# A fused attention, gated MLP and mixer kernel: tails transposed together, first loads on two queues, key sums moved up in each step

## The reference

```python
# attention with exponential features, per batch and head
def phi(x):
    proj = x @ w_phi                                   # 64 -> 128
    proj = proj - max(abs(proj), over features)
    return concat(exp(proj), exp(-proj))               # 256 features
kv  = phi(k).T @ v            # 256 x 64, a sum over all 576 keys
z   = sum over keys of phi(k)
out = (phi(q) @ kv) / (phi(q) @ z + 1e-6)
x   = heads side by side: 4 x 576 x 512
# gated MLP
h   = relu(x @ w_in)                                   # 512 -> 1024
c   = convolution of h over the sequence, 3 taps
x   = (h * sigmoid(c)) @ w_out                         # 1024 -> 512
# mixer
u   = x + (U V applied along the sequence, rank 32)
out = u + relu(u @ w_ch1) @ w_ch2                      # 512 -> 2048 -> 512
```

## Time and profile before

| | |
|---|---|
| median of 3 runs | 932.11 us (931.59 to 932.53) |
| the profiled execution | 931.04 us |
| its span, first to last instruction | 929.2 us |
| PE busy | 900.5 us, 97% |
| DVE, ACT, POOL busy | 377.8, 326.5, 90.9 us |
| granted TensorE clock, mean | 0.995 |

### The profile page before, as it was taken

How to read it: one execution, slowest core, us unless ns; L and a number is a source line. 1 busy time by engine, 2 the same in 40 slices (tenths; PEclk the granted TensorE clock), 3 DMA queues, 4 the chain that set the end, 5 groups by cost and what they waited for, 6 DMA issues and landing times.

```text
span 929.2 us, 14087 instructions
## 1 busy us (share of the span) xinstructions
PE 900.5 (97%) x5752; PEld 834.3 (90%) x5752; DVE 377.8 (41%) x655; ACT 326.5 (35%) x621; POOL 90.9 (10%) x60
## 2 busy tenths in 40 slices
PE   6899999999999999999998999999999999999997
PEld 4667889887988889889998999999999999999997
DVE  5455477226774355652595543221211122122111
ACT  5665565334653444543443332111211211211111
POOL 3323022000120001110042001010010010010000
PEclk9899999999999999999999999999999999999999
DMA  7986641304722236114356540110200300300101
GB/s 177 265 229 159 195 143 39 114 17 152 225 51 65 77 102 228 46 46 160 114 191 201 168 124 20 57 46 1 73 30 1 100 3 2 101 1 23 47 1 34
DMA packets 106032, 88.91 MB, mean 96 GB/s; under 512 B 61041, under 2 KB 92657, under 8 KB 103921
## 3 DMA queue, kind: packets, MB, share of 16 engines
q1 hardware_dynamic: 105968, 88.02, 31.6%
HBM read 70.18 MB, written 17.83 MB: 95 GB/s over the span
## 4 chain that ended last, share of the span: by engine, by line
PE 85%; DVE 4%; SPq 4%; DMA 3%; issue 2%; ACT 1%; ACTq 0%
PE qnb L1067 7%; PE qnb L1069 7%; PE qnb L1068 7%; PE qnb L1163 7%; PE mb L1067 6%; PE kvb L1124 6%; PE pjb L1067 5%; PE mb L1069 5%; PE mb L1068 5%; PE pjb L1069 5%; PE pjb L1068 5%; PE tpb L1067 2%; PE kvb L1069 2%; PE kvb L1067 2%; PE tpb L1068 2%
## 5 line engine op out<-in xcount | busy, mean ns | idle before, releaser
L985 DVE SCALAR_TENSOR_TENSOR c_lo<-qnb,c_hi 128x384 fp32r<-128x384 f32 x94 | 52.4, 558 | 284.9 <-ACT c_hi L752 284.9
L752 ACT ACTIVATE c_hi<-qnb 128x384 fp32r<-128x384 f32 x94 | 46.3, 492 | 296.6 <-PE qnb L1069 296.6
L1067 PE MATMUL qnb<-u_hi,w_b 128*128 128x384 f32 x384 | 129.8, 338 | 0.0
L1069 PE MATMUL qnb<-u_hi,w_b 128*128 128x384 f32 x384 | 128.4, 334 | 0.0
L1068 PE MATMUL qnb<-u_lo,w_b 128*128 128x384 f32 x384 | 128.4, 334 | 0.0
L809 DVE TENSOR_REDUCE nm<-pjb 128x4 f32<-128x512 f32 (+1 forms) x80 | 50.7, 633 | 84.5 <-PE pjb L1069 84.3
L508 POOL TENSOR_TENSOR g_lo<-cv,g_hi 128x576 fp32r<-128x576 f32 x32 | 48.2, 1505 | 361.5 <-DVE g_hi L794 361.5
L1067 PE MATMUL mb<-x_hi,winr 128*128 128x288 f32 x224 | 72.3, 323 | 0.1
L1067 PEld LDWEIGHTS qnb<-u_hi,w_b 128*128 128x128 f32 x384 | 72.1, 188 | 0.1
L1068 PEld LDWEIGHTS qnb<-u_lo,w_b 128*128 128x128 f32 x384 | 72.1, 188 | 0.0
L1069 PEld LDWEIGHTS qnb<-u_hi,w_b 128*128 128x128 f32 x384 | 72.1, 188 | 0.0
(11 more groups left out here) (257 smaller groups left out, 1929.2 us busy)
## 6 DMA issues: line engine op xcount, KB each, us to landing
winr<-wi_dram SPq DMA_DIRECT2D x32, 512.0 KB, 4.6
woutr<-wo_dram SPq DMA_DIRECT2D x15, 1024.0 KB, 5.9
stage<-in_moe_w_ch_dram SPq DMA_DIRECT2D x32, 256.0 KB, 4.6
us<-u_dram SPq DMA_DIRECT2D x6, 768.0 KB, 4.7
ua<-u_dram SPq DMA_DIRECT2D x6, 768.0 KB, 4.8
kr<-in_k_dram SPq DMA_DIRECT2D x32, 128.0 KB, 3.0
qr<-in_q_dram SPq DMA_DIRECT2D x32, 128.0 KB, 2.7
vt<-in_v_dram SPq DMA_DIRECT2D x32, 128.0 KB, 2.9
```

Of the source, the lines that this page charges most:

```text
L752: nc.scalar.activation(c_hi[:, j % CR, :], CH[j % 2][:, 0:TW], ACT.Relu).then_inc(s_chh, 1)
L985: nc.vector.scalar_tensor_tensor(out=c_lo[:, j % CR, :], in0=CH[j % 2][:, 0:TW], scalar=0.0, in1=c_hi[:, j % CR, :].bitcast(F32), op0=ALU. ...
L1067: mm(o, a_hi, b_hi, start=start, stop=False)
L1069: return mm(o, a_lo, b_hi, start=False, stop=stop)
```

## The change

1. The transposes of a tail move from step 5g - 1 to 5g - 3 (`T_TAIL`), and the transpose of the result's tail of pair g - 3 (`TAILS` = 3) goes into the same use of `TP`, in other columns: "p" is gone as a use of its own. A period has four uses ("q", "t", "k", "o") and one step without. ACT and DVE make both copies in one visit, with one count. Step -3 is now the first, and the tail of pair 0 the first use.
2. The first loads: SP issues q's tail, one half of k, both halves of q; ACT issues k's tail, the other half of k and both copies of w_phi, ahead of its first activation. The loads of q no longer stand behind SP's wait for the zeroed v.
3. The weight block c = 2 of the output product is loaded at m = 12 of SP's list where it was at m = 13.
4. PE: `contract_k` stands ahead of MLP piece 0, and `project` ahead of `kv_by_feature`. ACT: `key_values` stands ahead of `prepare_high`.
5. In batch 3 the low part of the last gated block is made by DVE, not POOL, with a semaphore of its own.
6. The first loads of u for the last product are issued among the loads of w_in of batch 3, and no longer wait for the store of batch 2's u.
7. `hidden2(1, 2)` stands ahead of the wait for the last four additions into u.

```diff
-    T_K, T_TAIL, T_Q, T_OUT, T_OUTT = -2, -1, 1, 10, 12
+    T_K, T_TAIL, T_Q, T_OUT, T_OUTT = -2, -3, 1, 10, 12
+    TAILS = (T_OUTT - T_TAIL) // PERIOD
...
     def tp_use(tick):
-        for kind, offset in (("o", T_OUT), ("q", T_Q), ("p", T_OUTT), ("k", T_K), ("t", T_TAIL)):
-            if here(tick, offset) is not None and (kind, here(tick, offset)) != ("p", NP - 1):
+        for kind, offset in (("o", T_OUT), ("q", T_Q), ("k", T_K)):
+            if here(tick, offset) is not None:
                 return kind, here(tick, offset)
-        return None
+        n, i = divmod(tick - T_TAIL, PERIOD)
+        return ("t", n) if i == 0 and 0 <= n < NP - 1 + TAILS else None
...
@@ SP, ahead of its list @@
-            load_k(0)
+            load_tail(0, QROWS, qd)
+            load_k(0, 0)
             for h in range(2):
-                sp.dma_start(ph_raw[h * D:(h + 1) * D, :], w_phi).then_inc(s_phi_ld, 16)
-            load_tail(0)
+                load_q(0, h)
             sp.wait_ge(s_zero, 2)
-            load_q(0)
             load_v(0)
...
@@ SP, weights @@
-                    if m in (13, 14):
-                        load_wout(b, m - 11)
+                    if m in (12, 14):
+                        load_wout(b, m // 2 - 4)
...
@@ SP, behind its list @@
             for j in range(WR, J1):
                 load_win(B - 1, j)
+                if j == J1 - 3:
+                    sp.wait_ge(s_xl, len(TPN))
+                    sp.wait_ge(s_ust, 16 * (B - 2))
+                    load_u(us, s_us, 0)
+                    load_u(ua, s_ua, 0)
             sp.wait_ge(s_u, 2 * CC * (B - 1))
             sp.dma_start(u_dram[:, :, (B - 2) * S:(B - 1) * S], x1[:, :, :]).then_inc(s_ust, 16)
-            sp.wait_ge(s_xl, len(TPN))
-            sp.wait_ge(s_ust, 16 * (B - 1))
-            load_u(us, s_us, 0)
-            load_u(ua, s_ua, 0)
...
@@ POOL @@
-            for n in range(J1 * B):
+            for n in range(J1 * B - 1):
                 gate_low(n)
...
@@ ACT, copies of the transposes @@
                 if kind == "t":
-                    act.wait_ge(s_pj, max(0, PERIOD * (g - 1) + TL + 1))
-                    copy(xl_hi[:, :], TP[:, 0:P]).then_inc(s_xh, 1)
+                    if g < NP:
+                        act.wait_ge(s_pj, max(0, PERIOD * (g - 1) + TL + 1))
+                        last = copy(xl_hi[:, :], TP[:, 0:P])
+                    if g >= TAILS:
+                        last = copy(x0_hi[:, (g - TAILS) % XS, MAIN:S], TP[:, P:P + TAIL])
+                    last.then_inc(s_xh, 1)
...
@@ ACT, ahead of its first activation @@
+            act.dma_start(tl[KROWS, 0, :, :],
+                          kd[0, 0, :, MAIN:S, :].rearrange("h s d -> s h d")).then_inc(s_tld[0], 16)
+            act.dma_start(kr[:, 0, :, 1, :],
+                          kd[0, 0, 1, 0:MAIN, :].rearrange("(p t) d -> p t d", t=TM)).then_inc(s_kld[0], 16)
+            for h in range(2):
+                act.dma_start(ph_raw[h * D:(h + 1) * D, :], w_phi).then_inc(s_phi_ld, 16)
             act.wait_ge(s_ident, 1)
...
@@ ACT, in a step @@
                 mlp(b, m, 1)
+                g = here(tick, 4)
+                if g is not None:
+                    key_values(g)
                 for n in range(NA):
                     if tick == prep_tick(n):
                         prepare_high(n)
-                g = here(tick, 4)
-                if g is not None:
-                    key_values(g)
...
@@ DVE, batch 3 @@
                     gate_high(b, j - 1)
+                if j == J1:
+                    dve.wait_ge(s_gh, J1 * B)
+                    sub(g_lo[:, J1 - 1, :], cv[:, (J1 * B - 1) % HR, :],
+                        g_hi[:, J1 - 1, :].bitcast(F32)).then_inc(s_glast, 1)
...
@@ PE, in a step @@
-                mlp(b, m, 0)
                 g, u = unit_at(tick - 2)
                 if g is not None and u <= TL:
                     contract_k(g, u)
+                mlp(b, m, 0)
                 mlp(b, m, 1)
-                g = here(tick, KVT0)
-                if g is not None:
-                    kv_by_feature(g)
                 g, u = unit_at(tick)
                 if g is not None:
                     if tick == 0:
                         pe.wait_ge(s_phi, 2)
                     project(g, u)
+                g = here(tick, KVT0)
+                if g is not None:
+                    kv_by_feature(g)
                 use = tp_use(tick)
...
@@ PE, ahead of the last product @@
+            hidden2(1, 2)
             pe.wait_ge(s_u, 2 * CC * B)
             for j in range(J2):
-                if j > 1:
+                if j > 2:
                     hidden2(1, j)
```

More of the change, by code:

```diff
@@ L57, in program @@
     MLP0 = PERIOD * (PAIRS - 1) + T_OUTT + 1
-    FIRST = T_K
+    FIRST = T_TAIL
     END = PERIOD * (NP - 1) + CQ0 + 2
@@ L109, in x0_use @@
     def x0_use(b):
-        return TPN["p" if b < B - 1 else "o", PAIRS * b + PAIRS - 1]
+        last = PAIRS * b + PAIRS - 1
+        return TPN["t", last + TAILS] if b < B - 1 else TPN["o", last]
     OUTS = [(c, h) for c in range(CC) for h in range(2)]
@@ L311, in _, with load_k, load_tail, load_q @@
                 sp.sem_inc(ahead, count)
[L313 to L329, removed]
+            def load_k(g, h):
+                sp.dma_start(kr[:, g % 2, :, h, :],
+                             kd[g // PAIRS, g % PAIRS, h, 0:MAIN, :].rearrange("(p t) d -> p t d", t=TM)
+                             ).then_inc(s_kld[g % 2], 16)
+            def load_tail(g, rows, src):
+                sp.dma_start(tl[rows, g % 2, :, :],
+                             src[g // PAIRS, g % PAIRS, :, MAIN:S, :].rearrange("h s d -> s h d")
+                             ).then_inc(s_tld[g % 2], 16)
+            def load_q(g, h):
+                sp.dma_start(qr[:, g % 2, :, h, :],
+                             qd[g // PAIRS, g % PAIRS, h, 0:MAIN, :].rearrange("(t p) d -> p t d", p=P)
+                             ).then_inc(s_qld[g % 2], 16)
             def load_v(g):
@@ L392, in _ @@
             sp.dma_start(cw[:, :, :], conv_w.rearrange("k (p j) -> p k j", j=J1)).then_inc(s_const_ld, 16)
-            load_k(1)
-            load_tail(1)
-            load_q(1)
+            for h in range(2):
+                load_k(1, h)
+            load_tail(1, QROWS, qd)
+            load_tail(1, KROWS, kd)
+            for h in range(2):
+                load_q(1, h)
             load_v(1)
@@ L412, in _ @@
                     sp.wait_ge(s_tp, TPN["k", g] + 1)
-                    load_k(g + 2)
+                    for h in range(2):
+                        load_k(g + 2, h)
                 g = here(tick - 1, T_TAIL)
@@ L416, in _ @@
                     sp.wait_ge(s_tp, TPN["t", g] + 1)
-                    load_tail(g + 2)
+                    load_tail(g + 2, QROWS, qd)
+                    load_tail(g + 2, KROWS, kd)
                 g = here(tick - 1, T_Q)
@@ L420, in _ @@
                     sp.wait_ge(s_tp, TPN["q", g] + 1)
-                    load_q(g + 2)
+                    for h in range(2):
+                        load_q(g + 2, h)
                 g = here(tick - 1, 4)
@@ L599, in transposed_high @@
                     last.then_inc(s_xh, 1)
-                if kind == "p":
-                    copy(x0_hi[:, g % XS, MAIN:S], TP[:, 0:TAIL]).then_inc(s_xh, 1)
             def query_features(g, half):
@@ L1083, in transposes @@
                 if kind == "t":
-                    pe.wait_ge(s_tld[g % 2], 32 * (g // 2 + 1))
-                    last = nc.tensor.transpose(TP[:, 0:P], tl[:, g % 2, :, :].rearrange("p h d -> p (h d)"),
-                                               ident[:, :])
+                    if g < NP:
+                        pe.wait_ge(s_tld[g % 2], 32 * (g // 2 + 1))
+                        last = nc.tensor.transpose(TP[:, 0:P], tl[:, g % 2, :, :].rearrange("p h d -> p (h d)"),
+                                                   ident[:, :])
+                    if g >= TAILS:
+                        last = nc.tensor.transpose(TP[:, P:P + TAIL], at[QROWS, (g - TAILS) % 2, TM, :],
+                                                   ident[QROWS, QROWS])
                 if kind == "o":
@@ L1093, in transposes @@
                         last = nc.tensor.transpose(KVT[:, 0:TAIL], at[QROWS, g % 2, TM, :], ident[QROWS, QROWS])
-                if kind == "p":
-                    last = nc.tensor.transpose(TP[:, 0:TAIL], at[QROWS, g % 2, TM, :], ident[QROWS, QROWS])
                 last.then_inc(s_tp, 1)
@@ L1197, in outputs @@
                         pe.wait_ge(s_wo[c % 2], woutr_loads(b, c))
-                if e == 0:
+                if e == 0 and (b, last) == (B - 1, J1):
+                    pe.wait_ge(s_gl, J1 * B - 1)
+                    pe.wait_ge(s_glast, 1)
+                elif e == 0:
                     pe.wait_ge(s_gl, J1 * b + last)
```

28 lines of the change are left out of this document (16 added, 12 removed).

## The result

The changed kernel takes 921.29 us as a median of 4 runs (919.92 to 921.39), the kernel before 931.85 beside it (930.87 to 932.53): a ratio of 0.9884, with a 95% interval from 0.9867 to 0.9901. The forecast was 920.2 with a range of 916.0 to 925.5. The profiled execution took 919.92 us, its span is 918.1; against the 929.2 of before that is 11.1 us less, where 11.85 was forecast. The other three runs are 1.4 us longer, at a mean clock of 0.997 or 0.998 where the profiled one had 0.999; what that may be is said at the end.

What follows compares the result with a forecast made beforehand. TensorE (PE) was taken as the bound, 85% of the chain of waits, with gains in its pauses and half-speed stretches. Terms summed to -11.85 us, 932.11 to 920.3; forecast 920.2, range 916.0 to 925.5.

Steps and rivals of the forecast that it cites:

- Part 4: Pair 1's period: copying key sums before ACT's split ends the 2.5 us wait, -4.5 us; PE's `project` swap, -0.5.
- Part 2: The start: k's transposes wait for DVE's split of w_phi, first projection at 9.5 instead of 7.97; +1.85 us in all.
- 0.45 for another operand: Start, step 3: ACT copies pair 1's tail only after a w_in split, delaying DVE's tail-feature difference, +0.45 us.
- Part 1: Tails sharing a bank use: PE's wait on k's low part goes; -1.8 us attention alone, -0.6 and -0.7 MLP stage.
- Part 3: Weight block c = 2 of the output product, loaded one step earlier, lands before its use: -2.4 us.
- Part 5: `contract_k` ahead of MLP piece 0 on PE: order alone gives 0 us (-0.4 to +0.4).
- Cover: MLP stage: without piece 0's 1.77 us in between, K0's features keep 0.57 us of margin; priced at 0.
- Part 6: End of batch 3: waits for the low part (-0.6), last weight block (-1.7) and additions (-0.9) go; -3.2 us together.

Runs made afterwards that it cites:

- b_load: The kernel before with only the first loads issued as in the changed kernel, every order the old one: 924.69 us beside 930.62.
- u_kv: The changed kernel with `key_values` back behind `prepare_high` on ACT: 918.40 us beside 931.21 for the kernel before.
- b_order: The kernel before with `contract_k` ahead of MLP piece 0 on PE as its one edit: 931.13 us beside 930.53.
- s_phi: The changed kernel with ACT issuing both copies of w_phi first, ahead of k's tail and half of k: 918.99 us beside 930.62 for the kernel before.
- u_wout: The changed kernel with weight block c = 2 of the output product loaded at m = 13 again: 924.96 us beside 930.62 for the kernel before.
- u_order: The changed kernel with `contract_k` back behind MLP piece 0 on PE: 919.47 us beside 931.21 for the kernel before.
- u_end: The changed kernel with the three edits at the end of batch 3 undone: 924.20 us beside 931.21 for the kernel before.
- best3: The changed kernel with `contract_k` behind piece 0, pair 0's tail low part ahead of w_phi's split, pair 1's loads ahead of U, V: 918.26 us beside 930.62.

## Why the prediction came out as it did

The time was right, and every wait that was to go went. One cause was wrong, its number right by luck, and the start was mis-sized.

**Part 4, the step that failed.** It forecast -4.5 us for pair 1's period from `key_values` ahead of `prepare_high` ("Now the copy goes first"). The period did fall by 4.47, but another edit does that alone. The first loads alone (b_load) take 4.9 us off that period with the old order, by a store that lands 3.1 us sooner; with them in, the new order gives nothing and costs 0.9 of the period (16.84 us against 15.96 in u_kv) and 0.6 in pair 0. The prediction held the piece it needed, "the store also goes out some 4 us earlier, since SP is ahead by 2.5 us", but as a side effect: it didn't ask what ACT's 2.99 us of idle time would be after that, and shorter queues on SP were priced at 0.15 us in part 2. Its bound of -2.3 to -5.2 was also made for one cause; two edits that would both remove the same wait should have been priced one at a time. Some of the 21.3 us was also the clock of that one execution: the same code took 19.94 in b_order. The 0.7 us by which the split holds up the query features was right at 42 us (a wait of 0.7); the same thing at 25 us, a wait of 1.4, was seen in part 2 only as 0.45 for another operand. The early `project`, as cover for `kv_by_feature`, was not tried alone, and neither was the sharing of the bank's use (part 1).

**Part 2, mis-sized.** +1.85 forecast, +2.86 measured: k's transposes at 7.69 (6.9), first projection at 10.31 (9.5), so 0.8 by w_phi, and the rest by the wait at 25 us. w_phi's two loads, issued at 2.27 and 2.96 on ACT, take 3.2 us to land where they took 2.3 to 2.6 on SP's queue alone, while loads of k and q are under way from SP; in s_phi, issued first, they take 2.1. This is what the Trainium skill states (DMA: Bandwidth & Descriptors, Issuing engines are not separate DMA queues): the second queue saves issue time, and the loads share the engines and interleave. The trace is in line with it, with 0.6 and 0.8 us more for the two loads; the prediction guessed 1 us from the rule and set it aside for want of a row. The place in a queue counts all the same: moving w_phi ahead won 0.9 us.

**Part 1.** Three periods of 0.6: -1.27 measured for pairs 2 to 4. L1172 waits 0.28 for the division (`at`) in each, as forecast. 0.88 less 0.28 is the forecast 0.6, and 0.42 a period came; the 0.18 between wasn't traced to an instruction. In the MLP stage the gains of parts 1 and 4 (forecast -0.6, -0.7 and -0.5) came to -1.1 in all, by the table's steps without those of part 3, one of the three losses of part 5 in it; in the mixing the waits of 0.56 of the tail are replaced by waits of L1240 on DVE, 1.1 us in two, so there next to nothing was won.

**Part 3.** -2.4 forecast, -2.5 measured (-1.44 and -1.02, two of the three losses of part 5 in them), by u_wout even more; b_load shows that 1.1 of the 2.4 us of waits would have gone by the loads alone.

**Part 5.** 0 (-0.4 to +0.4) forecast; the order costs 0.68 over the three batches by u_order against the profile after; the 0.6 between the medians of b_order can't be told from none. Cover was not the matter: K0's features are on time in every step. What the prediction didn't look at is the bank of the output product: with two pieces back to back the 1.5 us of key sums no longer lie between them while ACT empties it. That loses 0.27 in each of three batches, enough for all of it.

**Part 6.** -3.2 forecast; 0.77, 1.94 and 1.22 us at the three places, 3.9 in sum, and 4.05 when undone. Each was the size of its wait plus 0.1 to 0.3 of refill.

In sum: the start, part 1 and the MLP stage brought 1.0, 0.5 and 0.7 us less than forecast, the end 1.4 more (0.7 of that behind the last product, in the last store of the output, which comes with the first loads by b_load). The total is within 0.75 us of the profile because these cancel.

## What to carry to other kernels

When two edits could each remove the same wait, price each with the other undone; here the cheap one (four loads fewer at the head of a queue) did it alone, and with it in the visible reorder cost time. A shorter issue queue is worth what its latest consumer waits for: follow each wait on a DMA back to its issue, and from there up the queue to the start. A long piece of background work is best put in the time in which its engine would wait anyway, here even ahead of work with a nearer due time.

## What the hardware showed beyond expectation

- A pause of PE of 1.4 us around 25 us is followed by half clock in some executions and not in others. In the profiles of u_order and u_wout the stretch behind it (26 to 29.5 us) is at 0.50 to 0.66; in those of the changed kernel, u_end and s_phi it is at 1.00. The changed kernel's runs fall into 919.92 at a mean clock of 0.999 and three of 921.3 at 0.997 and 0.998, while u_kv, whose pause there is 0.6 us, has four runs within 0.25 us. best3, with the same pause, has two runs at 917.35 and 917.87 (0.999 and more) and two at 918.65 and 918.68 (0.998). That these belong together is argued from two profiles and the run clocks, not shown run by run.
- The 2.5 us wait of before cost 2.5 and, behind it, about as much again by the clock: b_load takes 4.9 us off the period with one edit. In b_order, the same code there, the wait was 2.0, the granted clock of the 6.7 us window 0.76 in place of 0.50, and the period 1.4 shorter. A wait of 1.9 us in u_wout cost 3.6.
- A 32 KB load of w_phi lands 2.1 to 2.2 us after its issue when it is first on ACT's queue (s_phi), 2.3 to 2.6 behind k on SP's (before), and 3.2 behind two loads on ACT's, with loads of k and q under way from SP (after). What is in flight beside it would explain this; it wasn't told apart from the place in the queue.
